# Reordering the elementwise chain of an attention and expert kernel, with its mask on the scalar engine, a per-head k by v product and logits from bf16 pieces

## What is computed

```python
# linear attention: 8 batches x 8 heads, 576 positions, head size 64
q_s = softmax(q, axis=-1)                  # per row of 64
k_s = softmax(k, axis=2)                   # per column, over the 576 positions
kv  = einsum('bhsd,bhse->bhde', k_s, v)    # 64 x 64 per head
x   = einsum('bhsd,bhde->bhse', q_s, kv)   # as 4608 rows of 512

# dense layer, 512 -> 2048 -> 512
h = x @ w_in
g = h - np.tanh(h)
y = g @ w_out

# 8 experts, each row goes to one: 512 -> 1024 -> 512
xn, en = y / |y|, expert_emb / |expert_emb|
logits = xn @ en.T / tau
expert = argmax(logits);  gate = softmax(logits)[expert]
out    = gate * (relu(y @ w1[expert]) @ w2[expert])
```

## Time and profile before

| what | value |
|---|---|
| median of 3 runs | 1539.16 us (1537.39 to 1543.4) |
| the profiled execution, its own time | 1541.91 us |
| its span in the trace | 1540.1 us |
| PE busy | 1463.5 us, 95% |
| PE weight load busy | 1273.6 us, 83% |
| DVE busy | 979.7 us, 64% |
| ACT busy | 639.8 us, 42% |
| POOL busy | 409.4 us, 27% |
| chain that ended last | PE 66%, DVE 20%, issue 7%, ACT 4% |

### The profile page before, as it was taken

How to read it: one execution, slowest core, us unless ns; L and a number is a source line. 1 busy time by engine, 2 the same in 40 slices (tenths; PEclk the granted TensorE clock), 3 DMA queues, 4 the chain that set the end, 5 groups by cost and what they waited for, 6 DMA issues and landing times.

```text
span 1540.1 us, 26303 instructions
## 1 busy us (share of the span) xinstructions
PE 1463.5 (95%) x7596; PEld 1273.6 (83%) x7597; DVE 979.7 (64%) x2003; ACT 639.8 (42%) x1268; POOL 409.4 (27%) x348
## 2 busy tenths in 40 slices
PE   4689999999999999999999999999999999999996
PEld 4577988989898988888888989997788888888885
DVE  7987678887777887867887786777422422342221
ACT  4454544555445554454554544444322323342220
POOL 3433233343324343423334332322000000101000
PEclk9899999999999999999999999999999999999998
DMA  8532011221101121101122000103711411411110
GB/s 183 158 88 85 1 44 26 59 54 32 39 8 45 40 68 41 51 3 45 31 53 54 17 21 8 69 15 103 249 61 41 150 41 41 151 36 48 42 38 25
DMA packets 139489, 90.87 MB, mean 59 GB/s; under 512 B 118872, under 2 KB 119128, under 8 KB 139232
## 3 DMA queue, kind: packets, MB, share of 16 engines
q1 hardware_dynamic: 132784, 70.12, 17.2%
q0 software_dynamic: 5840, 18.92, 3.2%
q10 hardware_dynamic: 736, 0.29, 0.1%
HBM read 70.39 MB, written 21.28 MB: 60 GB/s over the span
## 4 chain that ended last, share of the span: by engine, by line
PE 66%; DVE 20%; issue 7%; ACT 4%; DMA 1%; POOL 1%; SPq 0%; DVEq 0%; ACTq 0%; POOLq 0%
PE ps L513 19%; PE ps L514 19%; PE ps L515 19%; DVE gs L969 3%; DVE gs L966 3%; DVE big L964 2%; PE ps L689 2%; DVE gs L974 2%; PE ps L583 2%; PE ps L606 2%; DVE kfold L995 2%; DVE k_sb L1003 1%; DVE qrec L988 1%; PE ps L600 1%; PE ps L661 1%
## 5 line engine op out<-in xcount | busy, mean ns | idle before, releaser
L1348 POOL TENSOR_TENSOR g_lo<-gs,g_hi 128x384 fp32r<-128x384 f32 x192 | 216.8, 1129 | 324.5 <-ACT g_hi L773 324.0
L513 PE MATMUL ps<-x_hi,wi_hi 128*128 128x384 f32 x768 | 277.5, 361 | 0.0
L514 PE MATMUL ps<-x_lo,wi_hi 128*128 128x384 f32 x768 | 261.9, 341 | 0.0
L515 PE MATMUL ps<-x_hi,wi_lo 128*128 128x384 f32 x768 | 261.5, 340 | 0.0
L513 PE MATMUL ps<-wo_hi,g_hi 128*128 128x512 f32 x576 | 231.2, 401 | 14.8 <-POOL g_lo L1348 14.2
L514 PE MATMUL ps<-wo_lo,g_hi 128*128 128x512 f32 x576 | 230.0, 399 | 0.0
L515 PE MATMUL ps<-wo_hi,g_lo 128*128 128x512 f32 x576 | 228.4, 396 | 0.0
L773 ACT CAST g_hi<-gs 128x384 fp32r<-128x384 f32 x192 | 98.5, 513 | 293.2 <-DVE gs L974 292.8
L964 DVE TENSOR_SCALAR big<-usq 128x384 uint8<-128x384 f32 x192 | 115.3, 601 | 136.6 <-ACT usq L778 136.4
L883 ACT ACTIVATE hb<-ps 128x512 f32<-128x512 f32 x74 | 44.3, 599 | 305.2 <-PE ps L515 305.2
L513 PEld LDWEIGHTS ps<-x_hi,wi_hi 128*128 128x128 f32 x768 | 146.7, 191 | 3.6 <-issue 0.5
(11 more groups left out here) (200 smaller groups left out, 2746.7 us busy)
## 6 DMA issues: line engine op xcount, KB each, us to landing
w_raw<-w SPq DMA_DIRECT2D x10, 2048.0 KB, 9.2
xrow<-scratch SPq DMA_DIRECT2D x37, 257.0 KB, 2.7
q_sb<-q SPq DMA_DIRECT2D x62, 144.0 KB, 2.9
k_sb<-k SPq DMA_DIRECT2D x62, 144.0 KB, 3.3
v_sb<-v SPq DMA_DIRECT2D x60, 144.0 KB, 3.4
in_raw<-w_in SPq DMA_DIRECT2D x8, 512.0 KB, 5.7
out_raw<-w_out SPq DMA_DIRECT2D x8, 512.0 KB, 5.7
scratch<-pad_d SPq DMA_DIRECT2D x8, 257.0 KB, 4.6
```

The costliest lines, as they stand in the source:

```text
L513: mm(out_, a_hi, b_hi, start=first, stop=False)
L514: mm(out_, a_hi, b_lo, start=False, stop=False)
L515: return mm(out_, a_lo, b_hi, start=False, stop=last)
L1348: G.tensor_tensor(g_lo[:, (s - 1) % 3], gs[:, (s - 1) % 2], g_hi[:, (s - 1) % 3].bitcast(F32), ALU.subtract).then_inc(glo_ready, 1)
```

## The change

Five edits, the first two in the elementwise chain:

1. ACT makes `usq`, `th` and `gs` of chunk s first, and only then `g_hi` of chunk s-1.
2. The mask is made by ACT behind that, as relu(usq - 0.0625) in bf16, whose bits DVE's predicated copy reads as 16-bit integers. DVE's L964 is gone. `big` has one buffer instead of two.
3. The column maximum is spread over the rows by a transpose of `kmax` broadcast to 96 columns; `kdiag` (DVE) and the multiplication by ones are gone.
4. k by v is made per head: 12 matmuls 96 x 64 by 96 x 65 in place of 6 of 96 x 128 by 96 x 130. Head 0 writes partitions 0 to 63 of the bank, head 1 partitions 64 to 127. `v` has its column of ones behind each head.
5. Routing: the squares are summed by ACT. y is turned as before, but split into three bf16 pieces `y3`: ACT copies the first and the second, DVE makes the rest in PSUM and the third. The embeddings are split into three bf16 pieces `en3` once. The logits of a group are 12 bf16 matmuls with 24 columns, and DVE sums the three parts of each logit. The stages are a table now, `ROUTE`; place and scatter stand two stages later (stages 11, 12, 13). The twelfth block keeps the float32 logits and DVE's squares.

```diff
+ROUTE = {0: ("squares",), 1: ("norms", "turn:0"), 2: ("pieces:0",), 3: ("logits:0",), 4: ("turn:1",), 5: ("pieces:1",),
+         6: ("logits:1",), 7: ("turn:2",), 8: ("pieces:2",), 9: ("logits:2", "choose"), 10: ("ranks",),
+         11: ("dest", "scatter:0"), 12: ("scatter:1",), 13: ("scatter:2",), 15: ("stored",)}
...
-    big = sb("big", [P, 2, BLK], U8)
+    big = sb("big", [P, BLK], BF16)
...
 # PE
-                pe.wait_ge(kdiag_ready, u + 1)
-                mm(bankA[0:SP, 0:P], ones[:, 0:SP], kdiag_[:], start=True, stop=True).then_inc(maxrow_ready, 1)
+                pe.wait_ge(kmax_done, u + 1)
+                nc.tensor.transpose(bankA[0:SP, 0:P], kmax_[:, 0:1].broadcast_to([P, SP]),
+                                    ident[:]).then_inc(maxrow_ready, 1)
...
                 for r in range(R):
-                    last = mm(bankA[:, 0:VW], k_[:, r], v_[:, r, :], start=r == 0, stop=r == R - 1)
+                    for h in range(2):
+                        last = mm(bankA[h * HD:(h + 1) * HD, 0:HW], k_[:, r, h * HD:(h + 1) * HD],
+                                  v_[:, r, h * HW:(h + 1) * HW], start=r == 0, stop=r == R - 1)
...
+            elif what == "logits":
+                pe.wait_ge(ylo_ready, j * 3 + (g + 1))
+                for i in range(3):
+                    for dc in range(DC):
+                        last = mm(C[:, 0:3 * E], y3[:, i, dc * P:(dc + 1) * P],
+                                  en3[:, dc].rearrange("p i e -> p (i e)"), ...)
...
 # ACT, elementwise
-            if within(m, s, -1):
-                act.wait_ge(g_ready, done(m, s, -1))
-                act.wait_ge(l2_done, done(m, s, -4))
-                nc.scalar.copy(g_hi[:, (s - 1) % 3], gs[:, (s - 1) % 2]).then_inc(ghi_ready, 1)
             if within(m, s):
                 h = h_ps[s % 2][:, 0:BLK]
...
                 fn(gs[:, s % 2], usq[:, s % 2], ACT.Square, bias=cst[:, C_BIAS:C_BIAS + 1],
                    scale=SQ_SCALE).then_inc(s_ready, 1)
+            if within(m, s, -1):
+                act.wait_ge(g_ready, done(m, s, -1))
+                act.wait_ge(l2_done, done(m, s, -4))
+                nc.scalar.copy(g_hi[:, (s - 1) % 3], gs[:, (s - 1) % 2]).then_inc(ghi_ready, 1)
+            if within(m, s):
+                fn(big[:], usq[:, s % 2], ACT.Relu, bias=cst[:, C_SMALL:C_SMALL + 1]).then_inc(big_ready, 1)
...
 # ACT, routing
+            if what == "squares":
+                act.wait_ge(y_copied, j * 3 + 6)
...
+                for g in range(GPB):
+                    fn(C[:, 0:D], yrow[:, g, 0:D], ACT.Square, accum_out=ss[:, g:g + 1]).then_inc(ss_ready, 1)
...
+                nc.scalar.copy(y3[:, 0], C[:]).then_inc(yhi_ready, 1)
...
+                nc.scalar.copy(y3[:, 1], C[:]).then_inc(ymid_ready, 1)
...
 # DVE, elementwise
-            dve.wait_ge(u_ready, done(m, s))
-            V.tensor_scalar(big[:, s % 2], u, SMALL, None, ALU.is_ge).then_inc(big_ready, 1)
             dve.wait_ge(s_ready, done(m, s))
...
-            V.copy_predicated(g, big[:, s % 2], h).then_inc(g_ready, 1)
+            V.copy_predicated(g, big[:].bitcast(U16), h).then_inc(g_ready, 1)
...
 # DVE, attention and routing
-                dve.wait_ge(kmax_done, u + 1)
-                V.tensor_scalar(kdiag_[:], ident[:], kmax_[:, 0:1], None, ALU.mult).then_inc(kdiag_ready, 1)
...
+            if what == "turn":
+                dve.wait_ge(yhi_ready, j * 3 + (g + 1))
+                V.tensor_tensor(C[:], C[:], y3[:, 0], ALU.subtract).then_inc(yrest_ready, 1)
+            elif what == "pieces":
+                dve.wait_ge(ymid_ready, j * 3 + (g + 1))
+                V.tensor_tensor(y3[:, 2], C[:], y3[:, 1], ALU.subtract).then_inc(ylo_ready, 1)
```

More of the change, by code:

```diff
@@ L205, in unit_bufs @@
         if not isinstance(u, int) or u == 0 or u >= UPB:
[L206 removed]
+            return (q_sb[:, par], k_sb[:, par], v_sb[:, par], kvb[:, par], qT, kfold, qmax, qrec,
                     kmax, krec, A, Bk)
@@ L288, in route_at, with route @@
         return m * 3 + (s // FC1 - 1), s % FC1
+    def route(j, stage_, part):
+        for x in ROUTE.get(stage_, ()):
+            what, _, g = x.partition(":")
+            part(what, j, int(g or 0))
     def hold(eng):
@@ L616, in routing_stage @@
                 rows_turned(j, g, C)
-            elif stage_ in (3, 5, 7):
-                logits(j, g, C, yT)
-            elif stage_ == 8:
+            elif what == "logits":
[3 more added lines that the diff above has]
+                        last = mm(C[:, 0:3 * E], y3[:, i, dc * P:(dc + 1) * P],
+                                  en3[:, dc].rearrange("p i e -> p (i e)"), start=i == 0 and dc == 0, stop=i == 2 and dc == DC - 1)
+                last.then_inc(lg_ready, 1)
+            elif what == "ranks":
                 pe.wait_ge(oneh_ready, j + 1)
@@ L1400, in slot @@
             if at_:
-                routing_stage(*at_)
+                route(*at_, route_part)
         walk(pool, slot)
-        for st in range(14):
-            routing_stage(NBLK - 1, st)
+        route_part("norms", NBLK - 1, 0)
+        for g in range(GPB):
+            route_part("scatter", NBLK - 1, g)
         pool.wait_ge(tab_ready, 1)
```

143 lines of the change are left out of this document (80 added, 63 removed).

## The result

The change measured 1534.96 us (median of 18 runs, 1528.77 to 1540.79) against 1540.93 us for the kernel before (18 runs, 1536.66 to 1545.07). The ratio is 0.9962, 95% interval 0.9952 to 0.9973. I had forecast 1501, range 1478 to 1530. The change gained 6 us where I expected 38. The profiled execution took 1540.79 us, the highest of its runs; its span is 1539.0 us, so totals must not be compared by it, only stretches.

What follows compares the result with a forecast made beforehand. It took PE's own work plus its short waits as the bound. Terms -16 -3 -13 -7 -5 +5 +1 = -38 took the profiled 1541.9 us to 1504, a median near 1501; range 1478 to 1530.

Steps and rivals of the forecast that it cites:

- The expert stage, which the change leaves alone: Stage after the dense layer: expected not to move by more than 2 us; no term in the sum.
- Logits -16: Routing logits on PE: a group falls from 0.81 to 0.32 us, 33 groups, 16 us gained, all on PE's path.
- spread maximum -3: Spreading the column maximum on PE: one transpose pass replaces two passes, 0.11 us in each of 27 units, 3 us gained.
- k by v 0: k by v product on PE: 24 passes of 53 ns still take 1.26 us a unit, so no change.
- rival A: k by v: the two heads' array halves overlap, 0.63 us a unit, another 17 us gained, total 1484; chance 0.22.
- k waits -13: Routed slots: with squares off DVE, six PE waits of 2.2 us for k's exponential go, 13 us gained.
- clock -7: PE's half-clock stretches behind the waits for k, 17 us at 0.50, go with them; 7 us counted as gained.
- Early g_lo -5: Before 200 us: shorter DVE work removes half of PE's 9.8 us of waits for g_lo, 5 us gained.
- New g_lo +5: New PE waits for g_lo, mostly in a unit's last slot and where POOL's scatter waits for the rows' place: 5 us lost.
- DVE near 875: Sign to check: DVE's total busy time falls from 980 to near 875 us.
- B: Routed slots: only PE's work goes, ACT starts exponentials late and PE waits for k as before; total 1521, chance 0.19.
- D: Every attention unit: g_lo late by about 2.5 us, perhaps slowed beside DVE's operations; total about 1576, slower, chance 0.08.

Runs made afterwards that it cites:

- e1: The change plus 77 semaphore increments on DVE ahead of the expert loop, nothing else; 1515.17 us, ratio 0.9837.
- e2: The kernel before the change plus 27 semaphore increments on DVE ahead of the expert loop; 1559.35 us, ratio 1.0128.
- e13: e1 with the old logits put back (one float32 copy, eight float32 passes, no pieces); 1515.84 us, ratio 0.9836.
- e6: The changed kernel, padded as e1, with k by v made for both heads at once again; 1515.33 us, ratio 0.9836.
- e12: The kernel before with only the mask moved to ACT, ACT padded; 1534.45 us, ratio 0.9956.
- e8: The changed kernel, padded by 37 increments, with the squares of routing summed by DVE again; 1533.83 us, ratio 0.995.
- e9: The changed kernel, padded as e1, with a block's first scatter in stage 12 and the other two in stage 13; 1503.24 us, ratio 0.9747.
- e7: The changed kernel, DVE and ACT padded, with the mask made by DVE again; 1541.84 us, ratio 1.001.
- e4: e1 with ACT's g_hi put back ahead of the squares, tanh and gs; 1513.95 us, ratio 0.9833.

## Why the prediction was wrong

**"The expert stage, which the change leaves alone"** (may move by no more than 2 us) is the step that failed first. It moved by 25 us in the profiled execution, and its repair in e1 gives 20 of the 34 us between the forecast (1501) and the median (1535). The term had no number because I looked for the change's effect only where its lines are. e1 and e2 show what stood in its place: DVE's loop body is refetched in each pass or not, by where it begins (expert stage 503.7 and 496.1 us, or 478.5 and 478.6). With that repaired the change is at 1515 us, inside my range and 14 us above my forecast.

The rest by the terms of the sum, from e1 and the table of intervals:

- **Logits -16, spread maximum -3.** PE's own work fell as said (0.31 us a group). "All of it is on PE's path" was wrong: outside the k and scatter places the stretch from chunk 32 on gained 6.0 us, and e13 gives 0.7 us for the logits as a whole. I had argued PE to be the bound from a plain chunk; most logits stand in attention slots, whose end is set by DVE and POOL through `g_lo`.
- **k by v 0.** The size was 0.4 us a unit too high, the effect on the time right, for another reason: e6 shows the saving absorbed by the next wait. The halves don't run at the pace of rival A, and even at that pace, by e6, not all of the 17 us would have come. The Trainium skill's statement on overlapping halves ("TensorEngine Tiling (Array Packing)", Tiling Modes) fits only in part: 24 passes in 0.85 us are 35 ns each, 67% of the time I took for 65 columns, and a drain between halves shows in no row.
- **k waits -13, clock -7.** The waits went as said (13.1 us to 0.4 between 200 and 1040 us), and intervals 4 and 36 gained 24.6 us together. But the mask alone gives 5 to 7 of these in e12, and that the squares did the rest rests on the earlier trace rows; e8 brings back a wait of the same size at another place. The half clock behind these waits is gone; against "no 0.50 clock between 200 and 1040 us", two stretches of 3.4 us stand behind the scatter's wait instead (382.0 and 873.5 us), and a third begins at 1037.3. In e9 there is none between 200 us and 1008.
- **Early g_lo -5.** The first 32 intervals gained 8.0 us, and the mask alone gives as much in e12 (8.9). The wait that was to give it hardly moved: `g_lo` before 200 us went from 9.8 to 8.2 us. By which path the rest comes is not shown.
- **New g_lo +5.** The place was named ("where POOL's scatter waits for the place of the rows"), the size was not: 15.3 us. I had not noticed that the step moves from stage 9 to stage 11, into DVE's `kfold`. e9 takes it out.
- **DVE near 875.** 921 us; the multiplication, now mostly beside `g_lo`, takes 914 instead of 620 ns on average.
- **Not foreseen:** 6.4 us of waits for `y`, the third piece; and that without the mask's move the rest of the change gains nothing (e7, ratio 1.001, with some 4 us of it in the expert stage).

Of the rivals, B's total came near the truth of e1 by accident (1521 against 1515), but its mechanism, PE waiting for k as before, did not happen. Of D the late `g_lo` came, but at one place in two of three blocks instead of in each unit, at 1.6 to 2.0 us, and from the scatter's wait for the rows' place. The slowing that D named as a cause, DVE beside `g_lo`, came too, and in e4, where most of it is gone, the time is the same.

## What to carry to other kernels

Before costing a PE saving, ask slot by slot what ends the slot; the time from one product's start to the next, place by place, shows in one table what a saving is worth there and who takes it back. When instructions are moved off an engine, look at what stands behind them in the same program: the entry of a long loop (here 299 instructions) can move by a few dozen instructions and cost more than the edit gains. A step that waits (here the scatter on POOL) belongs in a slot where its producer is not behind something long, and not later than its buffer is needed.

## What the runs showed of the hardware

- DVE's code comes in packets of 8 KB on queue 14. A 299-instruction loop body stays loaded when it is entered at instruction 1443 or 1402, and is refetched when it is entered at 1327 or 1468, with DVE idle for up to 8.9 us in a pass and PE at the 1.2 GHz level behind the longer waits. Over the stage this is 18 to 25 us.
- The same multiplication of 128 x 384 float32 on DVE takes 639, 708 and 928 ns on average in three kernels: 0.53 to 0.56 us where it doesn't overlap POOL's subtraction, up to 2.3 us where it does.
- 24 passes with 64 weight columns and 65 columns in 0.85 us; 12 bf16 matmuls with 24 columns in 0.31 us.
- ACT's sum of squares of 128 x 512 costs two instructions, 603 ns and 189 ns for reading the accumulator.
